# All matmuls of TensorE in pieces of 256 columns, with g and its sums moved in SBUF

## What is computed

```python
scores = q @ pooled(k).T / sqrt(64)                  # 8 x 8 x 576 x 72
attn = softmax(scores); x = attn @ pooled(v)         # laid out as 4608 x 512
h = x @ w_in;  g = maximum(0.01 * h, h);             x = g @ w_out    # 512 -> 2048 -> 512
h = x @ w_in2; g = h * clip(h + 3, 0, 6) / 6;        out = g @ w_out2
```

## Time and profile before

| | |
|---|---|
| time, median of 3 | 1665.53 us (1662.83 to 1666.43) |
| profiled execution, its time | 1664.75 us |
| its span on the core | 1663.0 us |
| PE (matmuls) busy | 1652.8 us, 99% |
| PEld (weight loads) busy | 1500.9 us, 90% |
| DVE, ACT, POOL busy | 67%, 41%, 26% |
| DMA | 446.75 MB, 269 GB/s |
| matmuls | 11034 |

### The profile page before, as it was taken

How to read it: one execution, slowest core, us unless ns; L and a number is a source line. 1 busy time by engine, 2 the same in 40 slices (tenths; PEclk the granted TensorE clock), 3 DMA queues, 4 the chain that set the end, 5 groups by cost and what they waited for, 6 DMA issues and landing times.

```text
span 1663.0 us, 34820 instructions
## 1 busy us (share of the span) xinstructions
PE 1652.8 (99%) x11034; PEld 1500.9 (90%) x11034; DVE 1120.7 (67%) x2159; ACT 677.4 (41%) x1427; POOL 434.3 (26%) x451
## 2 busy tenths in 40 slices
PE   9999999999999999999999999999999999999998
PEld 7788888888888888889999999999999999999998
DVE  6768777686676867756455666676767676766665
ACT  5554443333332433333233544444444444444443
POOL 4346552021220212102336572021211111111100
PEclk9999999999999999999999999999999999999999
DMA  7746878678686786857779998898989898989884
GB/s 224 249 137 220 279 258 263 223 217 272 199 259 221 228 263 201 267 187 268 251 248 363 314 346 306 285 334 293 333 289 334 287 334 283 331 282 339 287 314 158
DMA packets 228499, 446.75 MB, mean 269 GB/s; under 512 B 23872, under 2 KB 48448, under 8 KB 219200
## 3 DMA queue, kind: packets, MB, share of 16 engines
q1 hardware_dynamic: 228416, 445.74, 79.4%
HBM read 379.58 MB, written 66.06 MB: 268 GB/s over the span
## 4 chain that ended last, share of the span: by engine, by line
PE 85%; DVE 0%; issue 0%; ACT 0%; DVEq 0%; ACTq 0%
PE ps_h L1734 38%; PE ps_y L1684 11%; PE ps_y L1685 11%; PE ps_y L1683 11%; PE ps_y L1819 5%; PE ps_att L1819 4%; PE ps_att L1856 2%; PE ps_att L1838 1%; PE ps_att L1684 1%; PE ps_att L1685 1%; PE ps_att L1683 1%; DVE xs_lo L1381 0%; DVE h L1412 0%; ACT y_stage L1132 0%; DVE gate L1348 0%
## 5 line engine op out<-in xcount | busy, mean ns | idle before, releaser
L1734 PE MATMUL ps_h<-xs_hi,ring 128*128 128x256 f32 x3808 | 810.4, 282 | 0.9 <-DVE h L1412 0.7
L1734 PEld LDWEIGHTS ps_h<-xs_hi,ring 128*128 128x128 f32 x3808 | 642.0, 189 | 31.7 <-issue 9.2
L1734 PE MATMUL ps_h<-xs_lo,ring 128*128 128x256 f32 x1904 | 533.2, 280 | 0.0
L1734 PEld LDWEIGHTS ps_h<-xs_lo,ring 128*128 128x128 f32 x1904 | 358.3, 188 | 17.0
L1097 ACT ACTIVATE g_hi<-gate 128x512 fp32r<-128x512 f32 x288 | 182.0, 632 | 376.3 <-DVE gate L1348 201.0
L1683 PE MATMUL ps_y<-g_hi,wout_hi 128*128 128x512 f32 x576 | 225.9, 392 | 0.6 <-DVE y_stage L1408 0.6
L1685 PE MATMUL ps_y<-g_hi,wout_lo 128*128 128x512 f32 x576 | 225.6, 392 | 0.0
L1684 PE MATMUL ps_y<-g_lo,wout_hi 128*128 128x512 f32 x576 | 225.4, 391 | 0.0
L1412 DVE TENSOR_TENSOR u<-ps_h,p 128x256 f32<-128x256 f32 x272 | 114.2, 420 | 123.2 <-PE ps_h L1734 107.6
L1089 ACT ACTIVATE pre<-h,three 128x512 f32<-128x512 f32 x144 | 103.2, 717 | 205.0 <-DVE h L1412 176.5
L1412 DVE TENSOR_TENSOR h<-ps_h,u 128x256 f32<-128x256 f32 x272 | 113.7, 418 | 56.4 <-PE ps_h L1734 54.5
(11 more groups left out here) (155 smaller groups left out, 2705.6 us busy)
## 6 DMA issues: line engine op xcount, KB each, us to landing
ring<-w_in_split SPq DMA_DIRECT2D x920, 256.0 KB, 3.7
w_sums<-w_out_sums SPq DMA_DIRECT2D x64, 1024.0 KB, 5.7
w_in_split<-ring SPq DMA_DIRECT2D x56, 256.0 KB, 3.9
w_in_split<-stage SPq DMA_DIRECT2D x56, 256.0 KB, 3.6
k_raw<-in_kT SPq DMA_DIRECT2D x32, 288.0 KB, 3.7
q_raw<-in_qT SPq DMA_DIRECT2D x32, 288.0 KB, 4.9
v_raw<-in_v SPq DMA_DIRECT2D x32, 288.0 KB
x0T<-x_stage SPq DMA_DIRECT2D x32, 288.0 KB, 3.5
```

What stands on the lines that cost most here:

```text
L1734: mm = pe.matmul(banks[BANK_OF[r]], a, b[:, r, c, :], start=r in OPENS and c == 0 and n == 0, stop=c == 1 and n == 2, skip_group_check=True)
```

## The change

A new helper, `product_by_halves`, takes the place of `product` for everything but the attention: it makes the three matmuls for columns 0 to 255 and then the three for 256 to 511, into the two halves of the same bank. The products of pairs and of `part` had 256 columns already. Attention's own shapes stay.

`g_hi` and `g_lo` now begin at a byte that is 64 modulo 256 in layer 1 (where they stream, and w_out at 128 is loaded) and 128 bytes later, at 192, in layer 2 (where they are loaded and w_out or `w_sums`, at 128, stream); `gs_hi` and `gs_lo` begin at 192. So in every product but the attention's what is loaded begins 64 bytes, modulo 256, behind what streams. Between kinds of product it is otherwise: while the last matmul of a run of ring and `xs` streams, the first weights of g for layer 2 are loaded, 128 behind, and while w_out streams the first of ring, level with it. Since the slots of layer 2 overlap the next slot of layer 1 by 128 bytes, ACT waits for one more use of g at the first three roundings of layer 2.

```diff
--- before.py
+++ after.py
@@ -100,6 +100,7 @@
 RING = 2 * PRODUCTS
 USES = HF * PRODUCTS // RING
 G_SLOTS = 4
+SECOND_AT = 32
 
 PIECES = 2 * GROUPS
 PIECE_GROUPS = (2, 0, 2, 0, 3, 1, 3, 1)
@@ -219,14 +220,19 @@
                 w_hi = sb(f"wout_hi{group}", [P, ROWS_IN, DM], F32R)
                 wout_raw[group] = overlaid(lambda sb: sb(f"wout_raw{group}", [P, ROWS_IN, DM]))
                 wout[group] = [w_hi, sb(f"wout_lo{group}", [P, ROWS_IN, DM], F32R)]
-        units[3] = overlaid(lambda sb: attention_buffers(sb, 3, 128))
+        units[3] = overlaid(lambda sb: attention_buffers(sb, 3, 448))
+        sb("before_p1", [P, 48])
         p1, u2, u3 = (sb(name, [P, HN]) for name in ("p1", "u2", "u3"))
         h = sb("h", [P, 2, N])
         gate = sb("gate", [P, 2, N])
         raw_s = overlaid(lambda sb: sb("raw_s", [P, 4, 2, P]))
         pre = sb("pre", [P, 2, N])
-        g_hi = sb("g_hi", [P, G_SLOTS, N], F32R)
-        g_lo = sb("g_lo", [P, G_SLOTS, N], F32R)
+
+
+        g_hi, g_lo = ([g[:, at:at + G_SLOTS * N].rearrange("p (s n) -> p s n", s=G_SLOTS)
+                       for at in (0, SECOND_AT)]
+                      for g in (sb("g_hi", [P, G_SLOTS * N + 2 * SECOND_AT], F32R),
+                                sb("g_lo", [P, G_SLOTS * N + 2 * SECOND_AT + 16], F32R)))
         x_stage = sb("x_stage", [P, DC, N])
         stage2 = overlaid(lambda sb: sb("stage2", [P, SLOTS2, 4, P], F32R))
         t_sum = sb("t_sum", [P, 4, 2, HN])
@@ -237,6 +243,7 @@
         def pair_buffers(sb):
             u = AttentionBuffers()
             u.w_sums = sb("w_sums", [P, 2, 4, DM], F32R)
+            sb("before_gs", [P, 16])
             u.gs_hi = sb("gs_hi", [P, 4, P], F32R)
             u.gs_lo = sb("gs_lo", [P, 4, P], F32R)
             u.gs = sb("gs", [P, 4, P])
@@ -1094,7 +1101,10 @@
                 n = 2 * s + 1 - upper
                 act.wait_ge(gate_ready, n + 1)
                 above_zero(act, g_used, n + 1 - G_SLOTS)
-                nc.scalar.activation(g_hi[:, g_slot(i, upper)], gate[:, upper], ACT.Copy,
+                if layer == 2 and isinstance(s, int) and n - 2 * HF * TILES in (0, 1, 2):
+
+                    act.wait_ge(g_used, n + 2 - G_SLOTS)
+                nc.scalar.activation(g_hi[layer == 2][:, g_slot(i, upper)], gate[:, upper], ACT.Copy,
                                      scale=1.0 / 6.0 if layer == 2 else 1.0
                                      ).then_inc(g_hi_ready, 1)
 
@@ -1360,12 +1370,12 @@
                 slot = (2 * i + 1 - upper) % G_SLOTS
                 dve.wait_ge(g_hi_ready, 2 * s + 2 - upper)
                 if layer < 2:
-                    nc.vector.tensor_tensor(g_lo[:, slot], gate[:, upper],
-                                            g_hi[:, slot].bitcast(F32), ALU.subtract
+                    nc.vector.tensor_tensor(g_lo[0][:, slot], gate[:, upper],
+                                            g_hi[0][:, slot].bitcast(F32), ALU.subtract
                                             ).then_inc(g_ready, 1)
                 else:
-                    nc.vector.scalar_tensor_tensor(g_lo[:, slot], gate[:, upper], 1.0 / 6.0,
-                                                   g_hi[:, slot].bitcast(F32),
+                    nc.vector.scalar_tensor_tensor(g_lo[1][:, slot], gate[:, upper], 1.0 / 6.0,
+                                                   g_hi[1][:, slot].bitcast(F32),
                                                    ALU.mult, ALU.subtract).then_inc(g_ready, 1)
 
             def piece_lo(piece):
@@ -1684,6 +1694,16 @@
                 pe.matmul(acc, left[0], right[1], start=False, stop=False)
                 return pe.matmul(acc, left[1], right[0], start=False, stop=last)
 
+            def product_by_halves(bank, left, right, first=True, last=True):
+
+                for half in range(2):
+                    cols = slice(half * HN, (half + 1) * HN)
+                    for n, (a, b) in enumerate(((0, 0), (0, 1), (1, 0))):
+                        mm = pe.matmul(bank[:, cols], left[a], right[b][:, cols],
+                                       start=first and half == 0 and n == 0,
+                                       stop=last and n == 2, skip_group_check=True)
+                return mm
+
             def keep_warm(count, bank):
 
                 for _ in range(count):
@@ -1701,8 +1721,9 @@
 
                     pe.wait_ge(x0_copied, 4)
                     pe.wait_ge(first_x_ready, chunk + 1)
-                mm = product(ps_h[:, upper, :], (w[:, d], w[:, 2 + d]),
-                             (xp_hi[:, chunk], xp_lo[:, chunk]), chunk == 0, chunk == DC - 1)
+                mm = product_by_halves(ps_h[:, upper], (w[:, d], w[:, 2 + d]),
+                                       (xp_hi[:, chunk], xp_lo[:, chunk]), chunk == 0,
+                                       chunk == DC - 1)
                 if chunk == DC - 1:
                     mm.then_inc(first_done, 1)
 
@@ -1750,11 +1771,12 @@
                 slot = (2 * i + 1 - upper) % G_SLOTS
                 cols = slice(j * P, (j + 1) * P)
                 if layer == 1:
-                    mm = product(ps_y[:, j, :], [w[:, row, cols] for w in wout[group]],
-                                 (g_hi[:, slot], g_lo[:, slot]), begins, ends)
-                else:
-                    mm = product(ps_y[:, j, :], (g_hi[:, slot, cols], g_lo[:, slot, cols]),
-                                 [w[:, row, :] for w in wout[group]], begins, ends)
+                    mm = product_by_halves(ps_y[:, j], [w[:, row, cols] for w in wout[group]],
+                                           (g_hi[0][:, slot], g_lo[0][:, slot]), begins, ends)
+                else:
+                    mm = product_by_halves(ps_y[:, j],
+                                           (g_hi[1][:, slot, cols], g_lo[1][:, slot, cols]),
+                                           [w[:, row] for w in wout[group]], begins, ends)
                 if j == DC - 1:
                     mm.then_inc(g_used, 1)
                 elif ends:
@@ -1806,7 +1829,7 @@
                 else:
                     slot = (2 * i + (r == A11)) % G_SLOTS
                     cols = slice(P, 2 * P) if r == A22 else slice(0, P)
-                    left = [g[:, slot, cols] for g in (g_hi, g_lo)]
+                    left = [g[1][:, slot, cols] for g in (g_hi, g_lo)]
                 if r in (A11, A12, S4):
                     group, row = divmod(i + HF * (r != A11), ROWS_IN)
                     cols = slice(HN, DM) if r == S4 else slice(0, HN)
```

## The result

The change makes the kernel slower: 1678.27 us (1677.30 to 1684.99, 5 runs) against 1664.57 (1662.83 to 1666.43, 5 runs), ratio of the means 1.0093, 95% interval 1.0071 to 1.0115 (the medians stand 0.8% apart). The forecast was 1657 and 1641 to 1672. The profiled execution took 1681.57 us, its span 1679.8, 16.8 more than the span in the earlier trace rows; it is 3.3 us above the median, so the tables by tile show somewhat more than the medians do.

A forecast was written before the change was run, and what follows sets the result against it. PE was taken as the bound: number of matmuls times distance between starts. Terms -9.6 - 1 + 0 + 1.8 + 0.5 gave -8.3 us, from 1664.75 to 1656.5, 1657.2 on the median's footing; forecast 1657, range 1641 to 1672.

The forecast's parts named there:

- the two beats: PE's 256-column matmuls start 113.3 ns apart (short) or 117.6 (long), kept until something with another stream moves it.
- Layer 2 in pairs: Tiles 10 to 17, 64 steps: 87 matmuls at the short beat, 9.97 us a step, a gain of 9.6 us.
- six crossings 0.07: Layer 2 steps: six passages between ring/xs and g tiles, 0.012 us each, bounds 0 and 0.03.
- Crossings that cost more than 0.03: Sign of being wrong: passing between pairs of tiles costs above the upper bound of 0.03 us.
- Tile 9: First tile of layer 2, 8 steps: 10.27 us a step against 10.39, a gain of 1 us.
- Tiles 7 and 8, zero, 3 us either way: Layer 1, 16 steps: 10.20 us short or 10.58 long against 10.39; 3 us either way, taken as 0.
- Tiles 1 to 6, a loss of 1.8: Layer 1 with attention, 48 steps: long beat short of everywhere, share taken as 0.6, a loss of 1.8 us.
- The waits added to ACT: Ahead of g_hi, first three half-steps of layer 2: covered, cost 0; uncovered, under 1 us once.
- g_hi waited for PE: Sign at the start of layer 2 that ACT's added wait is not covered.
- DMA: At 0.88 of its engines in a layer 2 tile; same bytes in 1.5% less time still fit, cost 0.
- Long beat in all of layer 1: Rival: each split product costs 8 ns more, 15 us lost, 1669, or 1676 with dear crossings; chance 0.12.
- The rival at 0.09: Rival by which the places of the tiles do nothing; chance 0.09.

The follow-up runs named there:

- split only: Kernel before with second products in pieces of 256, g and its sums at their old places, PE's loop over tiles 2 to 6 written out; 1679.32 us, 1.0092.
- the kernels without crossings: Kernel after with ring and xs 64 bytes further on in SBUF: with PE's loop written out 1671.46 us; with loop kept and layer 1 products whole 1660.19 us.
- Without the loop: Kernel after with PE's loop over tiles 2 to 6 written out, same matmuls, no jump; 1672.13 us, 1.0048.
- 24 whole: Kernel after, loop kept, 24 of a looped tile's 64 second products left as 512-column matmuls, a body of some 1660 instructions; 1672.68 us, 1.0049.
- before, no loop: Kernel before with PE's loop over tiles 2 to 6 written out; 1667.47 us, 1.0013.
- the third form of the added matmul: Added ahead of step 7 from tile 10 on, loading from 128, streaming from 64; the kernel, layer 1 whole plus three different added matmuls, took 1666.54 us, 1.0016.
- layer 1 whole: Kernel after with ring and xs 64 bytes further on in SBUF, layer 1 products whole at 512 columns, PE's loop kept; 1660.19 us, 0.9981.
- 384 idle waits: Kernel before with twelve already met waits at each place of PE's looped tiles, 384 more instructions, no added matmul; 1680.76 us, 1.0100.
- three distant matmuls a tile: Layer 1 whole plus one matmul loading from 128, streaming from 64, ahead of steps 1, 2 and 3 of tiles from 10 on; 1653.50 us, 0.9941.

## Why the prediction was wrong

**What bounds the kernel, the two beats, and how long they hold:** right for the most part. 113.3 and 117.6 ns were read from the earlier trace rows, and in layer 1 and between places 64 apart steady stretches show these two; level pieces of 256 settle at 120 (split only). The 9 in all 40 slices of the earlier trace rows is too coarse for one thing: in the kernel before too the granted clock is 0.50 from 58.2 to 61.3 us. And a whole matmul of 512 columns has two values too, 226 to 228 ns in the long beat and 230 to 233 in the short one (a quarter of those of layer 2 from tile 10 on), where the prediction had 227 for both.

**Layer 2 in pairs, "six crossings 0.07", 9.97 us a step:** the first step that failed; the step takes 10.18. The prediction took 0.68 us for a group of six L1842 and priced a crossing at 0.012 us, from one row behind a level crossing into ring; the new crossing from ring to g, 128 behind, had no row. It put all of the 0.03 that L1819 lost down to its level places. In the trace the group takes 0.71 as before, with places 64 apart, and the six of ring behind it 0.70. The tiles in the short beat throughout, in the kernels without crossings, show what 87 matmuls can take, 79.3 us; with crossings it is 81.67. That is 2.4 us a tile, 0.3 a step, 0.05 for each way from ring to g and back, four times my value and above my upper bound of 0.03. Taking the crossings away gives back only part of this by itself, since 8 of 14 tiles then ran long. Tiles 10 to 17 lost 5.5 us where 9.6 were to be gained. Crossings that cost more than 0.03 were rightly named as a sign of being wrong.

**Tile 9:** lost 1.7 instead of gaining 1, by the same term; its 48 pieces of w_out in each step come behind the crossing from ring.

**Tiles 7 and 8, zero, 3 us either way:** -0.3, with some luck: tile 7 ran short and tile 8 half short, half long. Without the loop the same two tiles took 1.8 more than before, with 24 whole 2.9, all within the bounds.

**Tiles 1 to 6, a loss of 1.8:** with the loop written out they gained 0.1, or 1.3 against the kernel before written out too; small as forecast, the sign not. The reason held in part. Behind pv0 the beat is short as forecast, but behind the scores it was short in two of the three cases from 454 to 505 us (0.68 for the six at 458.79 and 499.43, 0.71 for those at 478.78), and the first transposes left it long in both of theirs.

**The waits added to ACT:** without cost as predicted, though not covered as predicted: g_hi waited for PE, 4.3 us in all between 915 and 1015, which the prediction had named as the sign of it. No wait of PE for g appears. DMA: nothing lost, as predicted.

**What was missing altogether: the length of PE's program**, the second step that failed. No term priced 384 more instructions in a body that is run five times. They cost 8.2 us of stands and 6.3 of low clock by the windows, 12.2 in tiles 2 to 6 by the run without the loop. The page of the kernel before had a row to look at, 40 packets on q8. Beside the 61 of before, no loop, it shows a body that stays inside and is not fetched again; after the change it is the other way round, 88 with the loop and 79 without. By the runs a body of 1740 stays (no packet from 345 to 745 us) and one of 1804 does not (33 packets). Why the clock falls to 0.50 behind the stands was not shown.

Together: the prediction had -10.6 us for layer 2 and the trace has +7.2; it had +1.8 for tiles 1 to 6 and the trace has +12.7. These two make 29 of the difference of 25 between the spans and the sum; tiles 0, 7 and 8 go the other way by 3.5.

Of the rivals, none had the mechanism. "Long beat in all of layer 1" gave the right sign and, with dear crossings, nearly the time (1676), but its layer 1 did not come: tiles 1 to 6 without the loop lost nothing. The rival at 0.09, by which the places of the tiles do nothing, would have had the 0.71 of the L1842 groups right; the tiles at 79.3 us speak against it, in which the same matmuls from other places take 0.68.

What stays open: why the third form of the added matmul turns the beat, what in the array the two beats are, and why g's run stays long behind a crossing at 128. The runs show states and what moves them, not the machine behind them.

## What to carry to other kernels

Before splitting instructions inside a device loop, count the body, and look at the instruction queue's packets within the loop. Here a body of 1804 instructions on PE (33 packets from 345 to 745 us) cost some 2 us and a spell of over 3 us at a granted clock of 0.50 at every jump back, one of 1740 (no packet) nothing, in one execution. Price a change in many short runs by its transitions, not by the steady rate on either side of them: here 12 crossings a step cost 0.3 us against tiles in the short beat throughout, and undid a hoped-for gain of 0.2. Where the rate has two stable values, what sets it can be worth more than what it costs: three matmuls of 0.12 us a tile went with tiles of 79.9 us, where long ones take 82.3. Do not judge such a kernel by one profiled execution; compare the spread of its runs.

## What the runs showed of the hardware

- TensorE at a granted clock of 1.00, pieces of 256 columns: 113.3 or 117.6 ns from start to start, with the same instructions from the same tiles. Either was kept for hundreds of matmuls (690 of the long in layer 1 whole, 754 of the short from 764 us on in the kernel after). Where it changed in the stretches read here, it was at a wait, at another shape, or at a change of distance between what is loaded and what streams. Level pieces settle at 120 ns (split only).
- A loop body of 1420, 1660 or 1740 instructions on PE is kept between passes, without a packet (1740 in one execution); one of 1804 is fetched anew each time, with a stand of 1.9 to 2.3 us (2.5 to 3.4 with idle waits in it) at the jump and a granted clock of 0.50 behind it, 17 or 18 matmuls of 256 columns in 3.3 us, 0.21 us from start to start.
- The profile names the last semaphore, DVE's xs_lo, for stands that come with the length of PE's program (8.2 us in four waits at 1804 instructions, none at 1660 or without the loop). The kernel with 384 idle waits shows the same name with an unchanged DVE, and "issue" for one of its four.
- The best kernel found, layer 1 whole, layer 2 without crossings and with three distant matmuls a tile, takes 1653.50 us, 0.9941 (0.9927 to 0.9956) of the kernel before.
